# Attention and two feed-forward layers on one core: weights' preparation spread out, low parts of x moved between engines and groups, the last group's second products gathered at the end

## The reference, cut to what matters

```python
q_rot, k_rot = rotate(q), rotate(k)                 # q, k, v: (4, 8, 576, 64)
scores = scale * q_rot @ k_rot.T
attn = exp(scores - max) / (sum + 1e-9)
x = (attn @ v).transpose(0, 2, 1, 3).reshape(2304, 512)
h = x @ w_in1;  x   = (h - tanh(h)) @ w_out1        # w_in: 512 x 2048, w_out: 2048 x 512
h = x @ w_in2;  out = (h / (1 + exp(-h))) @ w_out2
```

## Time and profile before

| | us |
|---|---|
| median of 3 runs | 1045.99 (1045.75 to 1048.73) |
| the profiled execution | 1047.57 |
| its span | 1045.8 |
| busy: PE, weight loads, DVE, ACT, POOL | 1009.0, 921.0, 649.1, 528.1, 731.5 |
| attention, up to the first product L851 | 272.3 |
| the 48 groups and the end | 773.5 |

### The profile page before, as it was taken

The page is one execution under the profiler, slowest core; times in us unless marked ns, Lnnn a source line. Parts: engine busy times, 40 slices in busy tenths (PEclk is TensorE's granted clock), DMA queues, the critical chain, the costliest instruction groups (busy, mean ns, idle before and its releaser), DMA issues.

```text
span 1045.8 us, 17872 instructions
## 1 busy us (share of the span) xinstructions
PE 1009.0 (96%) x7116; PEld 921.0 (88%) x7116; DVE 649.1 (62%) x887; ACT 528.1 (51%) x791; POOL 731.5 (70%) x495
## 2 busy tenths in 40 slices
PE   3999999999899999999999999999999999999998
PEld 2889999999799998999989999888989889898897
DVE  6667677766555568556685466755676555764443
ACT  2667777877444354444453344543455443643432
POOL 6798999995475767756767767667668658587540
PEclk9999999999999999999999999999999999999999
DMA  5545565642212212212122122122121321223201
GB/s 178 182 124 182 153 193 158 196 141 64 56 41 81 81 42 81 64 57 81 42 81 81 41 81 80 42 81 75 47 81 42 141 81 55 67 87 107 69 21 60
DMA packets 68610, 94.56 MB, mean 90 GB/s; under 512 B 17328, under 2 KB 44208, under 8 KB 68528
## 3 DMA queue, kind: packets, MB, share of 16 engines
q1 hardware_dynamic: 68528, 93.43, 28.3%
HBM read 84.02 MB, written 4.79 MB: 85 GB/s over the span
## 4 chain that ended last, share of the span: by engine, by line
PE 86%; DVE 6%; POOL 3%; ACT 2%; DMA 1%; issue 1%; SPq 0%; ACTq 0%; DVEq 0%; POOLq 0%
PE ps L851 31%; PE ps L871 18%; PE ps L890 18%; PE ps L718 5%; PE ps L682 4%; PE ps L712 3%; DVE x_l L1170 2%; PE ps L620 2%; PE ps L684 1%; PE ps L672 1%; DVE hm L1102 1%; PE ps L748 1%; ACT th L1034 1%; ACT g_h L1041 1%; PE ps L638 1%
## 5 line engine op out<-in xcount | busy, mean ns | idle before, releaser
L548 POOL TENSOR_TENSOR win_l<-win_s,win_h 128x512 fp32r<-128x512 f32 x96 | 131.5, 1388 | 222.6 <-ACT win_h L974 222.6
L851 PE MATMUL ps<-x_h,win_l 128*128 128x384 f32 x672 | 227.4, 338 | 7.7 <-DVE hid L1218 4.5
L1034 ACT ACTIVATE th<-hid 128x768 f32<-128x768 f32 x96 | 80.5, 839 | 305.0 <-DVE hid L1218 305.0
L851 PE MATMUL ps<-x_l,win_h 128*128 128x384 f32 x672 | 227.6, 339 | 0.0
L851 PE MATMUL ps<-x_h,win_h 128*128 128x384 f32 x672 | 226.6, 337 | 0.0
L1218 DVE TENSOR_TENSOR hid<-ps,snap 128x384 f32<-128x384 f32 x192 | 106.3, 554 | 134.1 <-PE ps L851 133.3
L1102 DVE TENSOR_REDUCE hm<-ps 128x2 f32<-128x576 f32 x144 | 108.4, 756 | 59.4 <-PE ps L620 51.5
L851 PEld LDWEIGHTS ps<-x_h,win_l 128*128 128x128 f32 x672 | 126.6, 188 | 21.0 <-DVE hid L1218 6.4
L1218 DVE TENSOR_TENSOR snap<-ps,snap 128x384 f32<-128x384 f32 x144 | 79.5, 552 | 92.1 <-PE ps L851 92.1
L851 PEld LDWEIGHTS ps<-x_l,win_h 128*128 128x128 f32 x672 | 126.7, 189 | 10.6
L871 PE MATMUL ps<-g_h,wout_h 128*128 128x512 f32 (+1 forms) x384 | 129.9, 338 | 0.0
(11 more groups left out here) (100 smaller groups left out, 2153.0 us busy)
## 6 DMA issues: line engine op xcount, KB each, us to landing
win_s<-w_in SPq DMA_DIRECT2D x45, 512.0 KB, 4.9
wout_s<-w_out SPq DMA_DIRECT2D x45, 512.0 KB, 3.9
raw<-qk SPq DMA_DIRECT2D x30, 576.0 KB, 4.6
v<-vfull SPq DMA_DIRECT2D x16, 384.0 KB, 4.5
R<-inverse_sums SPq DMA_DIRECT2D x32, 144.0 KB, 3.1
vr<-vin SPq DMA_DIRECT2D x16, 192.0 KB, 3.4
out<-ostage SPq DMA_DIRECT2D x2, 1536.0 KB, 8.8
ev<-ev SPq DMA_DIRECT2D x16, 144.0 KB, 5.0
```

The costliest lines, as they stand in the source:

```text
L548: nc.gpsimd.tensor_tensor(lo, src, hi.bitcast(F32), ALU.subtract).then_inc(s_wl, 1)
L851: last = mm(ps[:, up_bank(g, i), 0:TH], a[w][:, BLOCKS[i], kk, :], b[i][:, kk, :], start=(k == 0), stop=(k == 5))
L1034: nc.scalar.activation(th[:, f, :], hid[g % 2][:, f, :], ACT.Tanh, scale=(1.0, 0.5)[g // (NT * NJ)]).then_inc(s_t, 1)
```

## The change

1. `W_LOAD`, `W_HIGH`, `W_SUMS`, `W_LOW`: the tables are drawn out. The four sums of group 0's blocks are made one a pair (pairs 3 to 6), those of group 1 all in pair 13; the high and low parts of the weights come one to three pairs later; the weights of group 2 are loaded in pairs 11 to 14, not 9 to 12.
2. POOL makes low parts 2 and 3 of the first tile in pair 15 ahead of `normalise(14)`. `normalise(15)` goes behind the weights of group 1, `invert(15)` on DVE behind the last gate's low part of group 0.
3. At each new tile, low part 3 goes from the last group of the old tile to the first of the new one, ahead of `add_product(g, 2)`; the x sum goes one place back; low part 6 goes from DVE to POOL, ahead of the low parts of the next group's weights.
4. In the last group, PE's chunks of second products stand 2, 1, 1, 1, 1, 6 behind products 1 to 6, not 3, 2, 1, 2, 1, 3.

```diff
         W_LOAD = {0: ("in", 0, 0), 1: ("in", 0, 1), 2: ("out", 0, 0), 3: ("out", 0, 1), 4: ("in", 1, 0), 5: ("in", 1, 1),
-                  6: ("out", 1, 0), 7: ("out", 1, 1), 9: ("in", 2, 0), 10: ("in", 2, 1), 11: ("out", 2, 0), 12: ("out", 2, 1)}
-        W_HIGH = {3: [(0, "A")], 5: [(0, "S01")], 6: [(0, "S23")], 7: [(0, "D")], 8: [(0, "O0")], 9: [(0, "O1")],
-                  11: [(1, "A")], 13: [(1, "S01")], 14: [(1, "S23"), (1, "D")]}
-        W_SUMS = {3: (0, 0), 4: (0, 1), 11: (1, 0), 12: (1, 1)}
-        W_LOW = {5: [(0, "A")], 6: [(0, "S01")], 7: [(0, "S23")], 8: [(0, "D")], 9: [(0, "O0")], 10: [(0, "O1")],
-                 13: [(1, "A"), (1, "S01")], 14: [(1, "S23"), (1, "D")]}
+                  6: ("out", 1, 0), 7: ("out", 1, 1), 11: ("in", 2, 0), 12: ("in", 2, 1), 13: ("out", 2, 0), 14: ("out", 2, 1)}
+        W_HIGH = {6: [(0, "A")], 7: [(0, "S01")], 8: [(0, "S23")], 9: [(0, "D")], 10: [(0, "O0")], 11: [(0, "O1")],
+                  12: [(1, "A")], 14: [(1, "S01"), (1, "S23"), (1, "D")]}
+        W_SUMS = {3: [(0, 0)], 4: [(0, 1)], 5: [(0, 2)], 6: [(0, 3)], 13: [(1, 0), (1, 1), (1, 2), (1, 3)]}
+        W_LOW = {7: [(0, "A")], 8: [(0, "S01")], 9: [(0, "S23")], 10: [(0, "D")], 11: [(0, "O0")], 12: [(0, "O1")],
+                 13: [(1, "A")], 14: [(1, "S01"), (1, "S23"), (1, "D")]}
...
-        X_POOL, X_DVE = (), (0, 1, 2, 3, 4, 6, 5)
+        X_POOL, X_DVE = (6,), (0, 1, 2, 4, 3, 5)
...
@@ POOL @@
-                if n >= PAIRS - 2:
-                    x_low(n - PAIRS + 2)
+                for i in {PAIRS - 2: (0,), PAIRS - 1: (1, 2, 3)}.get(n, ()):
+                    x_low(i)
                 if n >= 1:
                     normalise(n - 1)
-            x_low(2)
-            x_low(3)
-            normalise(PAIRS - 1)
             for g in range(1, GROUPS):
                 if g + 1 < GROUPS:
-                    weight_sums(g + 1, 0)
-                    weight_sums(g + 1, 1)
+                    for k in range(4):
+                        weight_sum(g + 1, k)
+                    if g % NJ == 0:
+                        x_low(6, tile_of(g))
                     for name in ("A", "D", "S"):
                         weight_low(g + 1, name)
                 weight_low(g, "O")
+                if g == 1:
+                    normalise(PAIRS - 1)
...
@@ PE @@
-                    for _ in range(((3, 2, 1, 2, 1, 3) if second else (2, 1, 1, 1, 1, 2))[i - 1]):
+                    for _ in range(((2, 1, 1, 1, 1, 6) if g >= GROUPS - 1 else (3, 2, 1, 2, 1, 3) if second else (2, 1, 1, 1, 1, 2))[i - 1]):
...
@@ DVE @@
             x_low(0, 6)
-            invert(PAIRS - 1)
...
                 if turn:
-                    x_sum(t, 3)
+                    x_low(t, 3)
                 add_product(g, 2, first, u2, 0)
                 if ahead:
                     x_low(t + 1, 1)
                 if turn:
-                    x_low(t, 6)
+                    x_sum(t, 3)
                 add_product(g, 3, u2, u3, 2)
                 if turn:
                     x_low(t, 5)
...
                 if ahead:
                     x_low(t + 1, 2)
-                if ahead:
-                    x_low(t + 1, 3)
                 add_product(g, 5, u3, h[:, 1, 0:TH], 3)
                 gate(g, 1)
                 add_product(g, 6, u4, h[:, 0, TH:TN], 5)
                 gate_low(g, 1)
+                if g == 0:
+                    invert(PAIRS - 1)
                 if ahead:
                     x_low(t + 1, 4)
```

More of the change, by code:

```diff
@@ L527, in normalise, with weight_sum @@
                                         ALU.mult).then_inc(s_xm, 1)
-            def weight_sums(g, part):
+            def weight_sum(g, k):
                 t = win_s[g % 2]
                 a11, a12, a21, a22 = t[:, 0:2, 0:128], t[:, 2:4, 0:128], t[:, 0:2, 128:256], t[:, 2:4, 128:256]
-                if part == 0:
+                if k == 0:
                     pool.wait_ge(s_wi[g % 2], staged(g))
@@ L536, in weight_sums @@
                         pool.wait_ge(s_wl, win_split(g - 1))
-                    nc.gpsimd.tensor_tensor(wsum[:, 0, :, :], a21, a22, ALU.add).then_inc(s_sc, 1)
-                    nc.gpsimd.tensor_tensor(wsum[:, 2, :, :], a11, a21, ALU.subtract).then_inc(s_sc, 1)
-                else:
[L540 to L543, removed]
+                else:
+                    pool.wait_ge(s_sc, 4 * g + (0, 1, 1, 3)[k])
+                o, a, b, op = ((0, a21, a22, ALU.add), (2, a11, a21, ALU.subtract), (1, wsum[:, 0, :, :], a11, ALU.subtract),
+                               (3, a12, wsum[:, 1, :, :], ALU.subtract))[k]
+                nc.gpsimd.tensor_tensor(wsum[:, o, :, :], a, b, op).then_inc(s_sc, 1)
             def weight_low(g, name):
@@ L581, in _ @@
                     rope_add(n + 3)
-                if n in W_SUMS:
-                    weight_sums(*W_SUMS[n])
+                for x in W_SUMS.get(n, ()):
+                    weight_sum(*x)
                 for x in W_LOW.get(n, ()):
                     weight_low(*x)
-                if n >= PAIRS - 2:
-                    x_low(n - PAIRS + 2)
+                for i in {PAIRS - 2: (0,), PAIRS - 1: (1, 2, 3)}.get(n, ()):
+                    x_low(i)
                 if n >= 1:
                     normalise(n - 1)
-            x_low(2)
-            x_low(3)
-            normalise(PAIRS - 1)
             for g in range(1, GROUPS):
                 if g + 1 < GROUPS:
-                    weight_sums(g + 1, 0)
-                    weight_sums(g + 1, 1)
+                    for k in range(4):
+                        weight_sum(g + 1, k)
+                    if g % NJ == 0:
+                        x_low(6, tile_of(g))
                     for name in ("A", "D", "S"):
```

## The result

The changed kernel takes 1051.12 us (median of 5 runs, 1050.93 to 1051.95); the kernel before, with more runs, 1045.75 (1045.11 to 1048.73). The ratio is 1.0051, interval 1.0037 to 1.0066: slower by half a per cent. The profiled execution of the changed kernel has a span of 1049.1 us and took 1051.1. The experiments ran in three batches on two chips, in which the kernel before takes 1047.8, 1046.6 and 1046.4 us; so their ratios to it, and lengths within the traces, can be compared, and medians from different batches only within some 2 us.

A forecast was written before the change was run, and what follows sets the result against it. It took PE to bound the kernel (86% of what ended last). The terms -3.0 - 4.4 + 12.0 - 0.7 = +3.9 us on the median of 1046.0 gave 1050, own range 1048.5 to 1053, widened to 1032.5 to 1053.

The forecast's parts named there:

- The turns: At five new-tile turns, GpSimd asks first and PE stalls 2.0 and 1.7 us; 12 us lost in sum.
- Part 1: In attention, weights spread over the pairs end ScalarE's late moves; gain 3.0 us, lower bound 2.4.
- Part 2: At the start of layer one, the first second product comes earlier; gain 4.4 us, bounds 2.9 and 5.1.
- Part 4: In the last group, an earlier add removes a wait and slow restart; gain 0.7 us, bounds 0.5 and 0.75.
- VectorE first: At the turns, VectorE's low part 3 goes before GpSimd's low part 6; 1034 us, chance 0.22.
- The second stall left out: At the turns, low part 5 slips in ahead of GpSimd's 1024-column piece; turns cost 3.5, 1041.4 us, chance 0.10.
- No hold at all: At the turns, GpSimd and VectorE do not hold each other; 1031.6 us, chance 0.05.
- Within 0.3%: Whole kernel: stalls shorter than forecast, or more gain at layer one's start; 1043 to 1049 us, chance 0.05.

The follow-up runs named there:

- before_again: The kernel before, unchanged, run once more: 1045.7 us.
- high6_later: The changed kernel with ScalarE's high part 6 moved behind the copy of the first weights' piece: 1043.34 us, ratio 0.9958 to the changed kernel's 1051.1... see text.
- turn_alone: The kernel before with only the new-tile edits (low part 3, low part 6, x sum): 1057.62 us, ratio 1.0109 to the kernel before.
- parts_124: The changed kernel with its turns as they were before: 1041.12 us, ratio 0.9936 to the kernel before.
- low6_halves: The changed kernel with GpSimd's low part 6 made by two instructions of 384 columns at the turns: 1042.99 us, ratio 0.9954.
- weights_halves: The changed kernel with GpSimd's 1024-column weights' pieces made by two instructions of 512 columns each, everywhere: 1044.15 us, ratio 0.9975.

## Why the prediction was right

**The turns.** Product 3 was forecast to wait 2.0 us, product 5 1.7 us, a turn 19.6 us in layer one and 19.3 in layer two. The chain gives 19.5 and 19.2, the sum is 97.1 against 85.6: +11.6 us, where 12 was forecast (11.0 against the execution of before_again). The order of asking was forecast with a lead of 0.1 us for GpSimd and is 0.09; low part 3 was forecast to take 2.7 and takes 2.60. The two waits are shorter than forecast: PE stands idle for 1.74 and 1.28 us, and counted from start to start of the matmuls about 1.9 and 1.4 are lost. The turn is as long as forecast all the same, as some 0.1 us more is lost at each restart and 0.3, not 0.1, at the group's first second product. high6_later turns the order round by moving one copy of 0.6 us ahead on ScalarE and takes 14.4 us off the turns. In all twelve traces, from layer one on, the order of the stamps decides when they are 0.05 to 0.3 us apart: VectorE's operations with both inputs in SBUF take 0.95 to 1.14 us in the 171 cases in which VectorE is stamped first, and 1.29 or more in the 102 in which GpSimd is. turn_alone and parts_124 show that the loss is in part 3 and needs no other part.

**Part 1.** Forecast -3.0. The two pairs went from 16.2 to 14.7 us each, 3.0 in sum. The first product of layer one came only 2.5 us earlier on the trace's clock, as the start of attention was 0.5 us later in this execution.

**Part 2.** Forecast -4.4 with bounds of 2.9 and 5.1. Against the execution shown before it is -4.9 (30.4 to 25.5 us for groups 0 and 1), against before_again -2.8 (28.3 to 25.5). The second is just below the lower bound. Here a size is off, by the execution that it was measured on: 2.1 us of what part 2 takes away there, of which 1.6 are PE at half clock, is not there in before_again or turn_alone (28.3 and 28.2 us for the two groups). The forecast had the half clock in its gain, at 1.5 us, and took the execution shown for the rule.

**Part 4.** Forecast -0.7; the stretch from the last group's start to the end went from 28.2 to 27.3, which is 0.9 and above the upper bound of 0.75.

**The sum.** +3.9 was forecast. The profiled executions differ by 3.3, the medians by 5.4; with before_again the difference of the spans is 5.1. Against before_again the terms are -2.2 for the attention (-3.0 forecast), -2.8 (-4.4), +11.0 (+12.0) and -0.9 (-0.7). Parts 1 and 2 gained 2.4 less than forecast, and the turns and the tail together cost 1.2 less; so the 1050 lies only 1.1 below the 1051.1 partly by luck, as misses of opposite sign cancel. It is within the forecast's own range of 1048.5 to 1053, and the mechanism is the one forecast.

**The rivals.** VectorE first (1034): high6_later is this case nearly, and took 1043. The rival's turns of 16.5 and 16.2 us are near the measured 16.65 and 16.35; it left out the group behind, where a later tie gives back 5.7 us. The second stall left out (1041.4): VectorE missed GpSimd's 1024-column piece by 0.44 us, not by 0.25. No run is this case; its turns would be 89.1 us (85.6 and 3.5), where low6_halves has 85.5, with a shorter first stall, and weights_halves 89.5. No hold at all (1031.6): the 2.60 us at 525.30 speak against it. Within 0.3%: the interval of the ratio begins at 1.0037.

What stays open: how the ties of a few hundredths of a us fall in the other executions of a kernel. The two traces of the kernel before have one that fell differently. Open too is the spread in the first pairs of attention: in the nine traces with the new tables the first product of layer one comes between 269.8 and 271.5 us, and most of this is there ahead of pair 3, the first in which the tables differ.

## What to carry to other kernels

Before work goes from VectorE to GpSimd, lay the two timelines side by side and ask for each pair of overlapping operations with all inputs in SBUF who asks first; a long GpSimd instruction ahead of a short VectorE one costs up to its whole length, though VectorE is busy for only 62% of the span and GpSimd for 70% in the kernel before. Let the engine on the path ask first, by ordering what feeds the other, and cut the other's long instructions in two: here both together turned a change that lost 0.5% into one that gains 1.1%. And carry such a replay one group past the place that is changed, since the next tie stands there.

## What the runs showed of the hardware that was not expected

The order is sharp: a lead of some 0.09 us was enough for GpSimd at all five turns, with VectorE's operations back to back, and one of 0.01 in high6_later (533.65 against 533.66). But at under 0.05 us the stamps can mislead: three gates with a lead of 0.01 to 0.04 us waited for a GpSimd sum of 0.7 us all the same. In the traces read here the hold stands in the instruction's own time, or as "issue" in the chain, and in no list of waits. Cutting the 1024-column pieces in two cost nothing that shows: the undisturbed groups keep their 629.3 us. And the kernel before has one trace with PE at half clock for 3.4 us behind two gaps of 1.9 and 1.2 us, and one with full clock behind gaps of 1.6 and 1.2. Whether the longer gap is the cause is not shown.
